# Two heads in one matmul: state product and keys by values on the whole 128x128 array

## The reference, cut to what matters

```python
for b in range(nb):
    qb, kb, vb = (q[:, :, sl], k[:, :, sl], v[:, :, sl])
    intra = np.einsum('bhic,bhjc->bhij', qb, kb) * Dmask[None]
    intra = np.einsum('bhij,bhjd->bhid', intra, vb)
    inter = np.einsum('bhid,bhde->bhie', qb * lam_pow[None], kv_state)
    out[:, :, sl] = intra + inter
    kv_state = lam_block[None, :, None, None] * kv_state + np.einsum('bhsd,bhse->bhde', kb * rev_pow[None], vb)
```

## Time and profile before

| | |
|---|---|
| median of 3 runs | 380.07 us (379.69 to 386.44) |
| the profiled execution, its own time | 379.69 us |
| its span, first to last instruction | 377.7 us |
| TensorE matmul / weight load busy | 356.3 us (94%) / 320.9 us (85%) |
| VectorE, ScalarE, GpSimd busy | 232.9, 176.8, 105.9 us |
| attention and routing | until about 90 us of the span |

### The profile page before, as it was taken

How to read it: one execution, slowest core, us unless ns; L and a number is a source line. 1 busy time by engine, 2 the same in 40 slices (tenths; PEclk the granted TensorE clock), 3 DMA queues, 4 the chain that set the end, 5 groups by cost and what they waited for, 6 DMA issues and landing times.

```text
span 377.7 us, 7035 instructions
## 1 busy us (share of the span) xinstructions
PE 356.3 (94%) x2680; PEld 320.9 (85%) x2680; DVE 232.9 (62%) x478; ACT 176.8 (47%) x304; POOL 105.9 (28%) x97
## 2 busy tenths in 40 slices
PE   7998999989999999999999999999997888969997
PEld 6877888779989989899898998989896776949786
DVE  6576888866471835819367292672705799883920
ACT  1235455311262735637355463554523684936342
POOL 4337998742000000000000000000017845443640
PEclk9999999958999999999999999999999999998999
DMA  7999997536148294773947739471017401001013
GB/s 229 418 414 401 401 406 302 168 104 192 39 153 295 111 328 127 270 274 115 325 157 266 248 123 348 142 271 62 0 62 204 129 1 57 28 28 57 2 56 113
DMA packets 30763, 70.13 MB, mean 186 GB/s; under 512 B 2320, under 2 KB 2832, under 8 KB 30224
## 3 DMA queue, kind: packets, MB, share of 16 engines
q1 hardware_dynamic: 26192, 59.25, 43.4%
q0 software_dynamic: 1920, 6.29, 5.1%
q10 hardware_dynamic: 2624, 4.22, 3.0%
HBM read 55.08 MB, written 14.68 MB: 185 GB/s over the span
## 4 chain that ended last, share of the span: by engine, by line
PE 70%; DVE 14%; DMA 8%; issue 3%; ACT 3%; POOL 1%; another core or an unknown queue 0%; SPq 0%; DVEq 0%; POOLq 0%; ACTq 0%
PE bank L1154 66%; DMA w_raw<-w 5%; DVE gate L1102 5%; DVE w_raw L1102 4%; DMA qkv_sb<-qkv 2%; PE bank L1312 2%; DVE x_all L1075 2%; PE bank L1212 1%; DVE w_sp L1067 1%; DMA x_all<-y_slots,gather_u 1%; POOL x_all L519 1%; ACT gate L749 0%; PE bank L1229 0%; DMA y_slots<-y_out 0%
## 5 line engine op out<-in xcount | busy, mean ns | idle before, releaser
L1154 PE MATMUL bank<-w_sp,h_sp 128*128 128x512 f32 (+1 forms) x480 | 106.4, 380 | 0.0
L1154 PEld LDWEIGHTS bank<-w_sp,h_sp 128*128 128x128 f32 x480 | 86.4, 188 | 16.4
L1154 PEld LDWEIGHTS bank<-x_sp,w_sp 128*128 128x128 f32 x768 | 93.2, 192 | 0.9 <-issue 0.3
L1154 PE MATMUL bank<-x_sp,w_sp 128*128 128x256 f32 x768 | 93.7, 283 | 0.1
L942 DVE TENSOR_TENSOR w_sp<-w_raw,w_sp 128x1024 fp32r<-128x1024 f32 x60 | 70.8, 1222 | 12.3 <-ACT w_sp L594 12.0
L594 ACT ACTIVATE w_sp<-w_raw 128x1024 fp32r<-128x1024 f32 x68 | 68.6, 1057 | 17.6 <-PE bank L1154 13.5
L519 POOL DMA_INDIRECT x_all<-y_slots,gather_u x12 | 12.6, 1052 | 194.5 <-DMA y_slots<-y_out 191.1
L1019 DVE SCALAR_TENSOR_TENSOR h_sp<-bank,h_sp 128x512 fp32r<-128x512 f32 x32 | 22.1, 690 | 63.6 <-ACT h_sp L634 62.6
L1154 PE MATMUL bank<-w_sp 128*128 128x384 f32 x192 | 37.0, 342 | 6.1 <-DVE prod L1117 3.2
L634 ACT ACTIVATE h_sp<-bank 128x512 fp32r<-128x512 f32 x32 | 19.1, 597 | 48.1 <-PE bank L1154 48.1
L1154 PEld LDWEIGHTS bank<-w_sp 128*128 128x128 f32 x192 | 32.9, 188 | 9.5 <-DVE prod L1117 4.3
(11 more groups left out here) (130 smaller groups left out, 418.6 us busy)
## 6 DMA issues: line engine op xcount, KB each, us to landing
w_raw<-w SPq DMA_DIRECT2D x32, 1024.0 KB
qkv_sb<-qkv SPq DMA_DIRECT2D x22, 512.0 KB, 12.7
x_slots<-zeros SPq DMA_DIRECT2D x4, 1024.0 KB, 15.3
x_in<-x_slots SPq DMA_DIRECT2D x7, 512.0 KB, 6.8
y_slots<-y_out ACTq DMA_DIRECT2D x7, 512.0 KB, 5.4
out<-x_in SPq DMA_DIRECT2D x11, 256.0 KB, 2.0
w_raw<-w_val SPq DMA_DIRECT2D x1, 1024.0 KB
w_raw<-w_out SPq DMA_DIRECT2D x1, 1024.0 KB
```

The costliest lines, as they stand in the source:

```text
L1154: return nc.tensor.matmul(o, lhsT, rhs, start=start, stop=stop, skip_group_check=free)
```

## The change

The two heads of a pair share one matmul. `state` and `state_dec` grow from [128, 2, 4, 64] to [128, 2, 4, 128]: for each pair a 128x128 matrix with the two heads' 64x64 states on its diagonal and zeros off it. GpSimd zeroes `state` once, ahead of `slot_iota` and `zeros`, and the first `add_state` waits for that. `between` issues 4 matmuls with 128x128 weights in place of 8 with 64x64; `keys_values` issues 4 with 128 columns in place of 8 with 64, and its blocks off the diagonal are not read. `add_state` becomes two instructions, one for each diagonal block, on 64 partitions each. `decay_state` is unchanged in the text, but its four instructions have 128 columns.

```diff
@@ -137,8 +137,8 @@
             q_scaled = sb_early("q_scaled", [P, 2, PAIRS, P])
             k_scaled = sb_early("k_scaled", [P, 2, PAIRS, P])
             scores_sb = sb_early("scores_sb", [P, 2, 2, PAIRS, P])
-            state = sb_early("state", [P, B, PAIRS, D])
-            state_dec = sb_early("state_dec", [P, B, PAIRS, D])
+            state = sb_early("state", [P, B, PAIRS, P])
+            state_dec = sb_early("state_dec", [P, B, PAIRS, P])
             xT = sb_early("xT", [P, 2, DT, P])
         x_in = sb("x_in", [P, 2, DM])
         x_sp = sb("x_sp", [P, 2, DT, CAP], F32R)
@@ -178,6 +178,7 @@
         q_decay_ok = sem("q_decay_ok")
         zeros_ok = sem("zeros_ok")
         warm_ok = sem("warm_ok")
+        state_zero = sem("state_zero")
         slots_zero = sem("slots_zero")
         dve_step = sem("dve_step")
         scaled_ok = sem("scaled_ok")
@@ -440,6 +441,7 @@
                            allow_small_or_imprecise_dtypes=True).then_inc(consts_ok, 1)
             nc.gpsimd.iota(iota_col[:, :], pattern=[[0, 1]], base=-1, channel_multiplier=CAP,
                            allow_small_or_imprecise_dtypes=True).then_inc(consts_ok, 1)
+            nc.gpsimd.memset(state[:, :, :, :], 0.0).then_inc(state_zero, 1)
             nc.gpsimd.iota(slot_iota[:, :], pattern=[[1, CAP]], base=0, channel_multiplier=0,
                            allow_small_or_imprecise_dtypes=True).then_inc(slot_iota_ok, 1)
             nc.gpsimd.memset(zeros[:, 2 * P:UNIT], 0.0).then_inc(zeros_ok, 1)
@@ -868,11 +870,16 @@
                 dve.wait_ge(kv_ok, t + 1)
                 if t >= B:
                     dve.wait_ge(decayed_ok, t - 1)
-                kv = ps_kv[:, 0:PAIRS * D].rearrange("p (a n) -> p a n", a=PAIRS)
-                if t >= B:
-                    nc.vector.tensor_tensor(state[:, b], kv, state_dec[:, b], ALU.add).then_inc(state_ok, 1)
-                else:
-                    nc.vector.tensor_copy(state[:, b], kv).then_inc(state_ok, 1)
+                elif t == 0:
+                    dve.wait_ge(state_zero, 1)
+                kv = ps_kv[:, :].rearrange("p (a n) -> p a n", a=PAIRS)
+                for s in range(2):
+                    r = slice(s * D, (s + 1) * D)
+                    if t >= B:
+                        last = nc.vector.tensor_tensor(state[r, b, :, r], kv[r, :, r], state_dec[r, b, :, r], ALU.add)
+                    else:
+                        last = nc.vector.tensor_copy(state[r, b, :, r], kv[r, :, r])
+                last.then_inc(state_ok, 1)
 
             def choose(t):
 
@@ -1173,10 +1180,7 @@
                 pe.wait_ge(state_ok, t - 1)
                 pe.wait_ge(xT_kept, t)
                 for a in range(PAIRS):
-                    for s in range(2):
-                        r = slice(s * D, (s + 1) * D)
-                        mm(ps_xT[r, a * P:(a + 1) * P], state[r, t % B, a, :], q_scaled[r, t % 2, a, :],
-                           a == 0, False, True)
+                    mm(ps_xT[:, a * P:(a + 1) * P], state[:, t % B, a, :], q_scaled[:, t % 2, a, :], a == 0, False, True)
 
             def keys_values(t):
                 pe.wait_ge(kv_in[t % RING], 16 * (t // RING) + 16)
@@ -1184,10 +1188,8 @@
                 if t:
                     pe.wait_ge(state_ok, t)
                 for a in range(PAIRS):
-                    for s in range(2):
-                        r = slice(s * D, (s + 1) * D)
-                        last = mm(ps_kv[r, a * D:(a + 1) * D], k_scaled[:, t % 2, a, r], qkv_sb[:, t % RING, 3, a, r],
-                                  True, True)
+                    last = mm(ps_kv[:, a * P:(a + 1) * P], k_scaled[:, t % 2, a, :], qkv_sb[:, t % RING, 3, a, :],
+                              True, True)
                 last.then_inc(kv_ok, 1)
 
             def within(t):
```

## The result

Over 20 runs of each, measured together, the changed kernel takes 381.94 us in the median (379.79 to 385.88) and the kernel before 379.62 (377.28 to 386.44). The ratio is 1.0065, with an interval of 1.0043 to 1.0089: slower by some 2.5 us. That is well within the 2% that were called the same, and inside the range; but the forecast was +0.2 us, and the interval excludes that. The profiled execution took 380.5 us.

The account below looks back on a forecast made before the run. Bound: the first expert weights' transfer and waits until 36.2 us, then busy TensorE to 73.8 us. Terms +0.64, +0.1 and -0.54 summed to +0.2 us; on the 380.07 us median it predicted 380.3 us, range 378.8 to 382.7.

Parts of the forecast that it names:

- the sum: Whole kernel: +0.64 us at tile 4, +0.1 over tiles 5 to 9, -0.54 for tiles 10 and 11, giving +0.2.
- likeliest case's own range: Whole kernel: 379.5 to 381.3 us, from unknowns of 0.3 us start, 0.2 state_dec and 0.1 a tile; chance 0.62.
- Steady tile: TensorE, tiles 2 to 9: four groups stay at 3.21 us, as three gaps saved offset 0.41 us more keys by values.
- The step that failed: TensorE's logits and state product: time beyond 0.11 us a record is shape-change gap, so new groups take 0.89 us each.
- Gaps belong to the change of shape, not to the waits: Between TensorE's groups: 0.10 to 0.15 us is lost where weight shape changes, none where shapes match despite a wait.
- Rival 2: TensorE's gaps belong to the waits, so keys by values costs 0.41 us a tile: +2.7 us, 382.8 us; chance 0.12.
- Rival 3: TensorE's state product and keys by values: half the instructions take half the time, -4.4 us, 375.9 us; chance 0.03.
- Tiles 10 and 11: TensorE's last two tiles, without keys by values: groups go from 2.59 to 2.32 us, saving 0.27 us each.
- rival 1: VectorE's two-half state update becomes the bound: 0.5 us more a tile, 3.0 on top, 383.3 us; chance 0.12.
- Restart at tile 4: TensorE's restart at 36.2 us: +0.44 us from the split update and 0.2 from four state_dec, +0.64 in all.
- The start costs nothing: GpSimd's new memset delays zeros by 0.9 us, but the load queue stays full: cost 0, at most 0.9 us.
- Rival 4: Slow clock between 80 and 90 us moves by 3 us: 1.5 us either way, 378.8 or 381.8 us; chance 0.11.

Follow-up runs that it names:

- e7: Changed kernel with keys by values back in 64-column pieces, plus six dummy matmuls before tile 4's logits; 378.79 us, ratio 0.9962 to the kernel before.
- e2: Changed kernel plus six dummy matmuls on zeros in TensorE's idle time before tile 4's logits; 379.88 us, ratio 1.0004 to the kernel before.
- e6: Kernel before with keys by values on 128 columns, update in two halves, state product still 64x64, six dummy matmuls at tile 4; 381.12 us, ratio 1.0047.
- e4: Changed kernel with the zeroing of state moved from GpSimd to VectorE; 384.5 us, ratio 1.0107 to the kernel before, from six runs.
- e3: Kernel before with only add_state split into two halves of 64 partitions, all matmuls as they were; 382.79 us, ratio 1.0048.
- e10: Changed kernel with the zeroing of state on VectorE plus six dummy matmuls at tile 4; 379.43 us, ratio 0.9986 to the kernel before.
- e1: Changed kernel run again with no edit, for a second trace; 383.70 us, ratio 1.0082 to the kernel before.
- e9: Kernel before with add_state split in two halves plus six dummy matmuls at tile 4; 380.24 us, ratio 1.0000 to the kernel before.
- e8: Kernel before plus six dummy matmuls at tile 4 and ten ahead of the routing behind the last tile; 377.46 us, ratio 0.9944.

## Why the prediction was right, and where its sum was not

The time lies in the range by the width that the rivals had given it, not by the sum. The likeliest case's own range, 379.5 to 381.3 us, does not hold the measured 381.94, and the change is worth +2.5 us where the sum had +0.2. The pace of the new shape, the gaps at changes of shape and the hiding of the longer update in the steady tiles came as worked out; 0.08 us in every tile, the restart and above all the clock did not.

**Steady tile, 3.21 us forecast as 3.21: measured 3.31.** Keys by values takes 0.89 and the transposes 0.53, as reckoned, and the logits 0.92, 0.03 over. The state product takes 0.97 instead of 0.89. The weight loads of the three groups start exactly 0.89 us apart (50.81, 51.70, 52.59), but a group's first record follows its load by 0.03 us behind the 9-column logits and by 0.11 behind a 128-column group. These 0.08 us are lost once, where narrow records give way to wide ones, with or without a change of shape; e7 shows them too (1.07 is 0.89 + 0.08 + 0.10). The step that failed took all of the old 0.99 + 1.02 beyond 8 x 0.11 for gaps of shape, by the earlier trace rows, where the wide group comes first and the narrow one second. With the 0.03 that is +0.40 us over four periods and +0.10 in the first tile (4.84 in e2 against 4.74), instead of the +0.1 charged for all of them.

**Gaps belong to the change of shape, not to the waits.** Right, and no longer only argued. In e7 the wait ahead of the state product stays and its gap goes, while the gap appears ahead of keys by values; in e6 both gaps stay. Rival 2 wanted 3.62 us (3.21 + 0.41) for the four groups. Rival 3 falls with it: the eight records of a group of the new shape take no less than 0.11 us each.

**Tiles 10 and 11, -0.27 each:** -0.18 each, by the same 0.08.

**VectorE.** 0.42 + 0.43 us without overlap, hidden in the steady tiles, as forecast; rival 1 falls, the strided halves cost nothing more. But the evidence was misread. The two `lam_pair` copies of the earlier trace rows were taken to be a first one of 0.46 us and a second one held behind it. The same view of the changed kernel (the two copies, and GpSimd's row beside them):

```profile
3.22 1.58 POOL L447 MEMSET zeros<- 128x1792 f32 x1
```

```profile
3.47 1.36 DVE L842 COPY lam_pair<-lam_all 64x4 f32<-64x4 f32 x1 [1.82 <-DMA lam_all<-lam]
```

```profile
4.84 0.17 DVE L842 COPY lam_pair<-lam_all 64x4 f32<-64x4 f32 x1
```

The first copy starts at the same 3.47 us and now lasts 1.36: it ends at 4.83, 0.03 behind GpSimd's memset at 4.80, as it ended 0.03 behind that memset's 3.90 before. It was blocked by GpSimd, not by its own length. In e4 the copies cost 0.62 us for both, with the memset back at its old time. The Trainium skill describes this ("SBUF — State Buffer", SBUF: two separate sides): VectorE and GpSimd share one pair of ports under an exclusive lock, which VectorE takes for some instructions only, an fp32 copy within SBUF among them, and whichever of the two starts second blocks fully. The trace agrees for this copy. That the halves of the update don't overlap is shown by the chain alone, 34.32 and 34.75.

**Restart at tile 4, +0.64: measured +1.05.** The two terms of the sum are there. The four `state_dec` cost 0.21 us (1.26 less 1.05), as charged. The second half of the update adds 0.44 (0.86 less 0.42), but the split costs 0.1 us more than that: the placing used to start 0.07 us ahead of the update's end and now starts 0.02 behind it. The sum took what follows the new update not to overlap it, but forgot that it had overlapped the old one. e3, the split alone, shows the same: its update starts at 33.84 and its placing at 34.73, 0.89 apart instead of 0.35, and its restart is 0.57 later (36.80). Another 0.26 us is the landing of the weights, and no run ties that to the change: ScalarE takes up the weights between 31.64 and 32.00 us in the six profiles of kernels with a compact state, and between 31.70 and 32.19 in seven of the eight with the wide one (in e10, behind its early fall, at 32.44). Without it the restart is +0.79.

**The start costs nothing.** Right, with a side effect that was not foreseen: through the blocked copy the keys are scaled at 8.89 us instead of 8.05 and tile 1's scores start at 12.16 instead of 10.73. At tile 4 it can't be told from the spread of the weights' landing, and e4 shows that taking it away brings TensorE's restart no nearer (37.25 against 37.28 and 37.15).

**The clock.** This is the term that the sum lacked. Rival 4 had the mechanism, even its price (half of some 3 us), but put it at 77 us alone and said "the change gives no direction". It may well: the sum's own +0.64 us at tile 4 is more idle time for TensorE ahead of 36 us, 1.4 to 1.7 us in place of 1.1, and all four profiles with that time left open (the changed kernel, e1, e3, e4) show the clock fall at 37.7 to 39.0 us. The kernel before does not, and of the nine kernels with dummies there none shows a fall between 35 and 76 us. Filling it is worth 1.0082 against 1.0004 (e1, e2; the intervals don't touch) and 1.0048 against 1.0000 (e3, e9; these touch). By the profiled executions the 2.83 us at the last routing are 1.64 for the fall, 0.93 for the change's own work in place of the forecast +0.2 (restart 0.79, first tile 0.10, periods 0.40, last two tiles -0.36), and 0.26 for the landing of the weights. That the first two add up to the 2.5 us of the timed executions is in part luck, as those show no stages.

**What stays open.** How often the fall comes in the timed executions of either kernel: only the profiled ones show where it lies. The mean clock doesn't tell: the changed kernel's in the first comparison is 0.9745, above the 0.9696 of e1 and equal to that of the kernel before in the comparison of e1 to e4. Nor is one fall all that divides e1 from e2, whose ratios are 3.0 us apart: e1's profile is at 0.66 of full speed from 290 to 300 us and at 0.83 from 340 to 350, and e2's at 1.00 in both. Whether these late falls follow from what happens at tile 4 isn't shown. Nor is what sets a fall off. Length of the idle time alone does not: e10 fell after 0.58 and 0.27 us, while the changed kernel's own profile has longer stretches with no fall behind them, 1.58 us ahead of 10.08 us and this one, with the clock at 1.00 from 340 to 350 us as shown above:

```profile
340.69 1.20 PE L1161 MATMUL bank<-w_sp,prod_sp 128*128 128x512 f32 x4 [3.35 <-ACT x_in L766]
```

And e4's 1.0107, which the longer fall in its profile would explain if it were the rule.

## What to carry to other kernels

A step that makes TensorE wait a few tenths longer can cost more than these tenths, as it did here at a wait that was already over a microsecond: look at the granted clock behind every long wait of the engine, before and after, and try dummy matmuls in it as an experiment. Fold small matmuls into whole-array ones only next to groups of that same shape, and count the gaps at changes of shape (0.10 to 0.15 us here) against the columns that the zeros add; the pairs of 64x64 pieces already ran side by side. When an instruction is split in two, count also the overlap that the next one had with it. And before a slow instruction is priced by its row, look at what the other engines did at the moment it ended.

## What the runs showed of the hardware that was not expected

- A tiny VectorE copy of 4 columns took 0.46 us in one kernel and 1.36 in the other, each time until GpSimd's memset ended, 0.17 when free.
- The granted clock fell to 1.2 GHz after TensorE had been idle for 1.4 to 1.7 us, and once after 0.58 and 0.27 us, but not after 3.35 us late in the changed kernel's profile. The fall cost 1.64 us at tile 4.
- With the fall behind the last tile taken away, 1.01 us of the gain turned at once into waiting for VectorE (e8).
- A group of eight 128-column records takes 0.97 us behind one of 9 columns and 0.89 behind one of 128.
